# Loading queries, keys and values for two pairs of heads per transfer, in an attention and two-layer expert kernel

## The chip, the cores and the metric

The kernel runs on one core of a Trainium2 chip. The metric is the device time of one execution in microseconds (us); lower is better. Before the change it is 928.75 us, the median of 3 runs (927.66 to 928.97).

## The reference

Everything is float32. Attention over q, k, v of shape 4 x 8 x 576 x 64 has two branches whose results are added: one over rows averaged in fours, one over a band of seven neighbours. The result, as 2304 rows of 512, goes through two layers with weights 512 x 2048 and 2048 x 512, the first with an ELU, the second with `s * relu(h)^2 + b`.

```python
q_d, k_d, v_d = (x.reshape(B, H, Sd, 4, D).mean(axis=3) for x in (q, k, v))
out_up = np.repeat(softmax_attn(q_d, k_d, v_d), 4, axis=2)
scores = np.where(abs(i - j) < 4, scale * q @ k.T, -1e9)
out_local = softmax(scores) @ v
x = (out_up + out_local).transpose(0, 2, 1, 3).reshape(B * S, H * D)
x = elu(x @ w_in0) @ w_out0
x = (s * relu(x @ w_in1) ** 2 + b) @ w_out1
```

## The kernel before

Two heads make a pair; there are 16 pairs (4 batches times CH = 4 pairs, called slots u), numbered i = 4n + u. Their arrays are laid out by the host: q and k with the head's 64 features ahead of the 576 positions, v with the two heads of a pair side by side.

The program has two stages. The **attention stage** takes the pairs one by one (`pairs` makes a loop over three batches and the fourth batch written out), and the **layers** then work through 6 blocks of 384 rows in each of two layers, with 16 chunks of weights each. Weights come through two staging buffers (`wstage`) and are split into a high and a low part by ScalarE (`hi_w`) and GpSimd (`lo_w`); the first four chunks of layer 0 are loaded and split during attention.

Within attention the engines run as a pipeline, each with its own written-out order, held together by counting semaphores. For pair i:

- SyncE (`sync`, L236) issues every load. `load_qk` (L238) is 3 transfers: keys of both heads into `kall[:, u]` (128 partitions), and each head's queries into its half of the partitions of `qbd`. `load_v` (L245) is 7 transfers: 9 overlapping windows of 70 rows into `vwin`, as six transfers in pieces of 512 B, and the rows grouped in fours into `v4` (in profile rows: `v`).
- TensorE (`tensor`, L418) in step i: pooled scores of i + 1 (`dscores`, L435), four of the transposes of i (`turn`, L450), the band scores of pair **i + 2** (`scores`, L426), the other transposes, and then `values` of i (L470, L479). It works strictly in this order, so a late query or key of i + 2 holds back the values of i.
- GpSimd (`gpsimd`, L324) in step i: pooled queries of pair **i + 3** (`pool_q`, L364, L366), pooled values of i + 1 (`pool_v`, L371, L373), and in slots 1 and 3 the low part of a chunk of weights (L378).
- ScalarE (`scalar`, L558) and VectorE (`vector`, L675): exponentials, copies out of PSUM, masks, maxima, normalisation. ScalarE also takes the high part of a chunk (L586) in step 1 and 3 of each batch, in the middle of its other work.

SyncE begins with q, k of pair 0, of pair 1, v of 0, q, k of 2, v of 1, q, k of 3, v of 2. Then `step` (L280) runs for each i: it waits until the scores and the pooled sums of i have been made, issues q and k of pair i + 4 into the same slot, in slot 0 issues two chunks of weights after waiting for the split of the chunks before them, then waits for the values of pair i - 1 and issues v of pair i + 3:

```python
if left >= CH:                       # q, k of pair i + 4
    sp.wait_ge(scores_ready, i + 1); sp.wait_ge(q_pooled, i + 1); sp.wait_ge(k_pooled, i + 1)
    load_qk(n + 1, u)
if u == 0:                           # two chunks of weights
    ...
if left >= 3:                        # v of pair i + 3
    sp.wait_ge(values_ready, i + 1)
    load_v(n + (u + 3) // CH, (u + 3) % CH)
```

(`values_ready` starts at 1.) Loads go to one queue and are served in the order of their issue.

Of the kernel before, what the change touches and what calls it, by code (L numbers as in the profile page):

```python
# [27 lines left out]
def attention_moe_moe2(nc, q_t, k_t, v, w_in0, w_out0, w_in1, w_out1, s, b, out):  # L28
    B, H, D, S = q_t.shape
# [34 lines left out]
    with ExitStack() as whole:  # L64
# [19 lines left out]
        with ExitStack() as first:  # L84
# [37 lines left out]
        q_loaded = [sem(f"q_loaded{i}") for i in range(CH)]  # L122
        k_loaded = [sem(f"k_loaded{i}") for i in range(CH)]
        v_loaded = [sem(f"v_loaded{i}") for i in range(CH)]
        w_loaded = [[sem(f"w_{x}_loaded{i}") for i in range(2)] for x in ("in", "out")]
        sb_loaded = sem("sb_loaded")

# [44 lines left out]
        block = whole.enter_context(nc.Block())  # L172

# [63 lines left out]
        def _(sp):  # L237
            def load_qk(bb, slot):  # L238
                sp.dma_start(kall[:, slot, :],
                             k_t[bb, 2 * slot:2 * slot + 2].rearrange("h d s -> (h d) s")).then_inc(k_loaded[slot], 16)  # L240
                for h in range(2):
                    rows = slice(h * D, (h + 1) * D)
                    sp.dma_start(qbd[rows, slot, h, :], q_t[bb, 2 * slot + h]).then_inc(q_loaded[slot], 16)  # L243

            def load_v(bb, slot):  # L245
                vp = v[bb, slot]
                inner = vp[QT - REACH:QT - REACH + (NT - 2) * QT].rearrange("(t r) x -> r t x", r=QT)
                rest = vp[2 * QT - REACH:2 * QT - REACH + (NT - 2) * QT].rearrange("(t r) x -> r t x", r=QT)
                dst = vwin[:, slot].rearrange("p t h d -> p t (h d)")
                sp.dma_start(dst[0:QT, 1:NT - 1, :], inner).then_inc(v_loaded[slot], 16)  # L250
                sp.dma_start(dst[QT:WIN, 1:NT - 1, :], rest[0:2 * REACH]).then_inc(v_loaded[slot], 16)
                for t in (0, NT - 1):
                    a = WSTART[t]
                    sp.dma_start(dst[0:QT, t, :], vp[a:a + QT]).then_inc(v_loaded[slot], 16)
                    sp.dma_start(dst[QT:WIN, t, :], vp[a + QT:a + WIN]).then_inc(v_loaded[slot], 16)
                sp.dma_start(v4[:, slot].rearrange("p k i x -> p k (i x)"),
                             vp.rearrange("(k p i) x -> p k (i x)", k=2, i=POOL)
                             ).then_inc(v_loaded[slot], 16)
# [66 lines left out]
        def _(pool):  # L325
# [35 lines left out]
            def pool_q(n, u):  # L361
                pool.wait_ge(q_loaded[u], 32 * (n + 1))
                x = qbd[:, u].rearrange("p h (a i) -> p (h a) i", i=POOL)
                pool.tensor_tensor(q_half[:, u % 2], x[:, :, 0:2], x[:, :, 2:4], ALU.add).then_inc(q_part, 1)  # L364
# [3 lines left out]
            def pool_v(n, u):  # L368
                pool.wait_ge(v_loaded[u], 16 * NV * (n + 1))
                x = v4[:, u]  # L370
# [48 lines left out]
        def _(pe):  # L419
            def scores(n, u):  # L420
                pe.wait_ge(k_loaded[u], 16 * (n + 1))
                pe.wait_ge(q_loaded[u], 32 * (n + 1))
                for t in range(NT):
                    bank, a = (0, t * WIN) if t < NTA else (1, (t - NTA) * WIN)
                    for h in range(2):
                        mm = pe.matmul(ps_s[h * QT:(h + 1) * QT, bank, a:a + WIN], qbd[:, u, h, t * QT:(t + 1) * QT],  # L426
# [32 lines left out]
            def values(n, u):  # L459
                i = n * CH + u  # L460
                slot = u % 2
                pe.wait_ge(v_loaded[u], 16 * NV * (n + 1))
                pe.wait_ge(x_ready, i + 1)

                def band_tiles(tiles):
                    for t in tiles:
                        for h in range(2):
                            rows = slice(h * D, (h + 1) * D)
                            o = ps_x[rows, 0, t * QT:(t + 1) * QT] if t < NTA else ps_x[rows, 1, (t - NTA) * QT:(t - NTA + 1) * QT]
                            mm = pe.matmul(o, vwin[:, u, t, h, :], probt[:, t, h * QT:(h + 1) * QT], start=True, stop=True)  # L470
# [373 lines left out]
```

## Time and profile before

| | |
|---|---|
| median of 3 runs | 928.75 us |
| the profiled execution: its own time | 932.17 us |
| its span, first to last instruction | 930.4 us |
| attention stage | 0 to about 125 us of the span |
| TensorE busy over the span | 905.8 us (97%) |
| bytes read from HBM | 36.09 MB |

The span is 1.8 us shorter than the execution's own time, and that is 3.4 us over the median of the three runs. Times in rows count from the start of the span. A busy engine is an engine with an instruction under way; "idle before" gives the time an instruction's engine stood still and what released it. "SPq" is SyncE's issuing of transfers.

### The profile page before, as it was taken

What the parts mean: (1) busy time and instruction counts of PE and PEld (TensorE: products, weight loads), DVE (VectorE), ACT (ScalarE), POOL (GpSimd) and SP (SyncE); (2) the same over time, 40 slices, a digit from 0 to 9 for tenths busy, and PEclk for the clock granted to TensorE, in tenths of its full rate; (3) what the DMA queues carried; (4) which work ended last, traced back from release to release, by engine and by line L of the source; (5) the groups of instructions that cost most, each with busy time, mean ns of one, the idle gap of its engine ahead of it and who ended that gap; (6) DMA issues with size and microseconds to landing.
All of it is one profiled execution on the core that took longest, in us unless ns stands there. A gap on an engine that the chain in (4) does not pass through costs nothing.

```text
span 930.4 us, 16164 instructions
## 1 busy us (share of the span) xinstructions
PE 905.8 (97%) x5936; PEld 853.6 (92%) x5936; DVE 396.3 (43%) x774; ACT 413.1 (44%) x1104; POOL 148.3 (16%) x148
## 2 busy tenths in 40 slices
PE   5898999999999999999999999999999999999998
PEld 5777789999999999999999989899998999999896
DVE  6788844233233233232333453443443443443433
ACT  8889976544344343344466432232232332322222
POOL 5565647300000000000156400000000000000000
PEclk9889999999999999999999999999999999999999
DMA  8987534200000000000044200000000000000000
GB/s 196 206 199 195 131 100 135 62 1 1 1 0 0 0 0 0 0 1 1 23 125 125 69 1 0 35 1 1 35 0 0 34 0 0 35 1 1 34 1 35
DMA packets 42929, 41.47 MB, mean 45 GB/s; under 512 B 3616, under 2 KB 30080, under 8 KB 42880
## 3 DMA queue, kind: packets, MB, share of 16 engines
q1 hardware_dynamic: 42880, 40.83, 16.7%
q8 instruction: 30, 0.49, 0.2%
q14 instruction: 19, 0.16, 0.1%
HBM read 36.09 MB, written 4.72 MB: 44 GB/s over the span
## 4 chain that ended last, share of the span: by engine, by line
PE 90%; SPq 2%; issue 2%; POOL 2%; DVE 2%; ACT 1%; DMA 1%; POOLq 0%; ACTq 0%; DVEq 0%
PE ps_h L517 43%; PE ps_y L538 22%; PE ps_y L536 21%; PE ps_t L450 1%; PE ps_sd L435 1%; POOL v L371 1%; SPq L243 1%; PE ps_xd L479 1%; PE ps_s L426 1%; ACT prob L568 1%; DMA wstage<-in_w_in 1%; PE ps_x L470 1%; DVE prob L700 0%; POOL q_half L364 0%; POOL qd L366 0%
## 5 line engine op out<-in xcount | busy, mean ns | idle before, releaser
L660 ACT ACTIVATE g_hi<-tmp 128x384 fp32r<-128x384 f32 x192 | 101.0, 526 | 262.5 <-PE ps_y L538 153.1
L654 ACT ACTIVATE tmp<-ps_h 128x384 f32<-128x384 f32 x192 | 94.2, 490 | 227.2 <-PE ps_h L517 224.7
L804 DVE TENSOR_TENSOR g_lo<-tmp,g_hi 128x384 fp32r<-128x384 f32 x192 | 107.4, 559 | 205.4 <-ACT g_hi L660 205.4
L517 PE MATMUL ps_h<-xs_hi,win_late_lo 128*128 128x384 f32 x576 | 193.8, 336 | 0.0
L517 PE MATMUL ps_h<-xs_hi,win_late_hi 128*128 128x384 f32 x576 | 193.8, 336 | 0.0
L517 PE MATMUL ps_h<-xs_lo,win_late_hi 128*128 128x384 f32 x576 | 193.6, 336 | 0.0
L796 DVE SCALAR_TENSOR_TENSOR tmp<-tmp,ps_h 128x384 f32<-128x384 f32 x96 | 53.2, 554 | 162.1 <-ACT tmp L657 161.2
L517 PEld LDWEIGHTS ps_h<-xs_lo,win_late_hi 128*128 128x128 f32 x576 | 108.3, 188 | 3.3
L517 PEld LDWEIGHTS ps_h<-xs_hi,win_late_hi 128*128 128x128 f32 x576 | 108.3, 188 | 3.2
L517 PEld LDWEIGHTS ps_h<-xs_hi,win_late_lo 128*128 128x128 f32 x576 | 108.3, 188 | 0.0
L800 DVE TENSOR_TENSOR tmp<-tmp 128x384 f32<-128x384 f32 x96 | 55.2, 575 | 121.1 <-ACT tmp L654 121.1
L536 PE MATMUL ps_y<-g_hi,wout_late_lo 128*128 128x384 f32 x288 | 96.8, 336 | 0.0
L536 PE MATMUL ps_y<-g_lo,wout_late_hi 128*128 128x384 f32 x288 | 96.8, 336 | 0.0
L536 PE MATMUL ps_y<-g_hi,wout_late_hi 128*128 128x384 f32 x288 | 96.8, 336 | 0.0
L538 PE MATMUL ps_y<-wout_late_hi,g_lo 128*128 128x512 f32 x216 | 85.2, 394 | 0.0
L538 PE MATMUL ps_y<-wout_late_lo,g_hi 128*128 128x512 f32 x216 | 85.0, 394 | 0.0
L538 PE MATMUL ps_y<-wout_late_hi,g_hi 128*128 128x512 f32 x216 | 84.9, 393 | 0.0
L517 PE MATMUL ps_h<-xs_hi,win_early_hi 128*128 128x384 f32 x192 | 64.7, 337 | 0.2 <-DVE xs_lo L749 0.2
L517 PE MATMUL ps_h<-xs_hi,win_early_lo 128*128 128x384 f32 x192 | 64.4, 335 | 0.0
L517 PE MATMUL ps_h<-xs_lo,win_early_hi 128*128 128x384 f32 x192 | 64.3, 335 | 0.0
L378 POOL TENSOR_TENSOR win_early_lo<-wstage,win_early_hi 128x512 fp32r<-128x512 f32 (+1 forms) x8 | 10.2, 1280 | 292.3 <-ACT win_early_hi L586 292.3
L536 PEld LDWEIGHTS ps_y<-g_lo,wout_late_hi 128*128 128x128 f32 x288 | 54.1, 188 | 0.0
(87 smaller groups left out, 1435.9 us busy)
## 6 DMA issues: line engine op xcount, KB each, us to landing
wstage<-in_w_in SPq DMA_DIRECT2D x32, 256.0 KB, 2.8
wstage<-in_w_out SPq DMA_DIRECT2D x32, 256.0 KB, 2.8
kall<-in_kt SPq DMA_DIRECT2D x16, 288.0 KB, 4.4
qbd<-in_qt SPq DMA_DIRECT2D x32, 144.0 KB, 4.2
v<-in_v SPq DMA_DIRECT2D x16, 288.0 KB
out<-wstage SPq DMA_DIRECT2D x18, 256.0 KB, 2.2
vwin<-in_v SPq DMA_DIRECT2D x16, 224.0 KB
vwin<-in_v SPq DMA_DIRECT2D x32, 32.0 KB
```

Source lines behind the costliest of these rows:

```text
L243: sp.dma_start(qbd[rows, slot, h, :], q_t[bb, 2 * slot + h]).then_inc(q_loaded[slot], 16)
L371: pool.tensor_tensor(x[:, :, 0:2, :], x[:, :, 0:2, :], x[:, :, 2:4, :], ALU.add).then_inc(v_part, 1)
L378: pool.tensor_tensor(lo, wstage[slot][:, half, :], hi.bitcast(F32), ALU.subtract).then_inc(w_split[half], 1)
L426: mm = pe.matmul(ps_s[h * QT:(h + 1) * QT, bank, a:a + WIN], qbd[:, u, h, t * QT:(t + 1) * QT], kall[:, u, WSTART[t]:WSTART[t] + WIN], sta ...
L517: mm = pe.matmul(o, w_chunk(0, a, j)[:, c * P:(c + 1) * P], xs[x][:, slot, c, :], start=(c == 0 and p == 0), stop=(c == CH - 1 and p == 2))
L536: mm = pe.matmul(ps_y[:, c, 0:TB], w_chunk(1, a, j)[:, c * P:(c + 1) * P], g[x][:, j % 2, :], **go)
L538: mm = pe.matmul(ps_y[:, c, 0:DM], g[a][:, j % 2, c * P:(c + 1) * P], w_chunk(1, x, j), **go)
L654: act.activation(x, ps_h[:, j % 4, 0:TB], ACT.Relu, scale=-1.0 if layer == 0 else 1.0).then_inc(relu_ready, 1)
L660: act.activation(g[0][:, j % 2, :], x, ACT.Copy).then_inc(hi_ready, 1)
L796: dve.scalar_tensor_tensor(out=x, in0=x, scalar=-1.0, in1=ps_h[:, j % 4, 0:TB], op0=ALU.add, op1=ALU.max).then_inc(act_ready, 1)
L800: dve.tensor_tensor(x, x, x, ALU.mult).then_inc(square_ready, 1)
L804: dve.tensor_tensor(g[1][:, j % 2, :], x, g[0][:, j % 2, :].bitcast(F32), ALU.subtract).then_inc(g_ready, 1)
```

## The change

Two pairs (slots 2g and 2g + 1) form a group. The host lays q, k and v out so that what a group needs of one partition lies together, and each transfer now brings both pairs: runs of 4608 B in place of 2304 B for q and k, 1024 B in place of 512 B in the windows of v, 4096 B in place of 2048 B in `v4`. There is one semaphore for each group's q, k and v in place of one for each slot. Pairs 0 and 1 alone still get q and k in transfers of their own, with two extra semaphores for pair 0. The other loads of q and k and all loads of v go by groups: the first ones come in the order q, k of 0; q, k of 1; v of 0 and 1; q, k of 2 and 3; v of 2 and 3. In `step`, q, k of the next batch's group are issued in slots 1 and 3 only (pairs i + 3 and i + 4), and so is v (the same two pairs, after the values of pair i).

```diff
-            qbd = sba("qbd", [P, CH, 2, S])
+            qbd = sba("qbd", [P, 2, CH, S])
             kall = sba("kall", [P, CH, S])
-            vwin = sba("vwin", [WIN, CH, NT, 2, D])
-            v4 = sba("v4", [KD, CH, 2, POOL, 2 * D])
+            vwin = sba("vwin", [WIN, CH // 2, NT, 2, 2, D])
+            v4 = sba("v4", [KD, CH // 2, 2, POOL, 2, 2 * D])
...
+        def wait_q(eng, n, u):
+            if isinstance(n, int) and n == 0 and u == 0:
+                eng.wait_ge(first_q_loaded, 32)
+            else:
+                eng.wait_ge(q_loaded[u // 2], 32 * (n + 1))
...
-            def load_qk(bb, slot):
-                sp.dma_start(kall[:, slot, :],
-                             k_t[bb, 2 * slot:2 * slot + 2].rearrange("h d s -> (h d) s")).then_inc(k_loaded[slot], 16)
+            def load_qk(bb, grp, a, z):
+                slots = slice(2 * grp + a, 2 * grp + z)
+                k_done, q_done = (first_k_loaded, first_q_loaded) if z == 1 else (k_loaded[grp], q_loaded[grp])
+                sp.dma_start(kall[:, slots, :], k_t[bb, grp, :, a:z, :]).then_inc(k_done, 16)
                 for h in range(2):
                     rows = slice(h * D, (h + 1) * D)
-                    sp.dma_start(qbd[rows, slot, h, :], q_t[bb, 2 * slot + h]).then_inc(q_loaded[slot], 16)
+                    sp.dma_start(qbd[rows, h, slots, :], q_t[bb, grp, h, :, a:z, :]).then_inc(q_done, 16)
...
-            load_qk(0, 0)
-            load_qk(0, 1)
+            load_qk(0, 0, 0, 1)
+            load_qk(0, 0, 1, 2)
             load_v(0, 0)
-            load_qk(0, 2)
+            load_qk(0, 1, 0, 2)
             load_v(0, 1)
-            load_qk(0, 3)
-            load_v(0, 2)
...
             def step(n, u, left):
                 i = n * CH + u
-                if left >= CH:
+                if left >= CH and u % 2 == 1:
                     sp.wait_ge(scores_ready, i + 1)
                     sp.wait_ge(q_pooled, i + 1)
                     sp.wait_ge(k_pooled, i + 1)
-                    load_qk(n + 1, u)
+                    load_qk(n + 1, u // 2, 0, 2)
                 if u == 0:
                     for half in range(2):
                         sp.wait_ge(w_split[half], n + 1)
                         load_w(0, n, half, 0)
-                if left >= 3:
-                    sp.wait_ge(values_ready, i + 1)
-                    load_v(n + (u + 3) // CH, (u + 3) % CH)
+                if left >= CH and u % 2 == 1:
+                    sp.wait_ge(values_ready, i + 2)
+                    load_v(n + 1, u // 2)
```

The consumers change only in their indices and in the semaphore they wait for.

**Order on SyncE, the first loads.** Each row is one instruction: its line, and the tile it fills with the shape (partitions first). Before, the loads of v of pair 0, q and k of pair 2, and the beginning of v of pair 1:

```order
L256 DMA v<-in_v 72x2x512
L239 DMA kall<-in_kt 128x576
L243 DMA qbd<-in_qt 64x576 x2
L250 DMA vwin<-in_v 64x7x128
L251 DMA vwin<-in_v 6x7x128
```

Now, the same place:

```order
L275 DMA v<-in_v 72x2x1024
L259 DMA kall<-in_kt 128x1152
L262 DMA qbd<-in_qt 64x1152 x2
L269 DMA vwin<-in_v 64x7x256
L270 DMA vwin<-in_v 6x7x256
```

The transfers are as many, and each is twice as large; the queries and keys of pair 2 stand behind the values of two pairs, and are complete only with those of pair 3.

**Order on SyncE, the first step of the loop** (`ISA` stands for register work and waits, `wstage` for a chunk of weights). Before, after the last of the first loads:

```order
L278 DMA sb<-in_b 128x1
L176 UNCONDITIONAL_BRANCH
L176 ISA
L239 ISA
L239 DMA kall<-in_kt 128x576
L243 DMA qbd<-in_qt 64x576
L243 ISA
L243 DMA qbd<-in_qt 64x576
L264 ISA
L264 DMA wstage<-in_w_in 128x4x128
L264 ISA
L264 DMA wstage<-in_w_out 128x512
```

Now:

```order
L295 DMA sb<-in_b 128x1
L192 UNCONDITIONAL_BRANCH
L192 ISA
L283 ISA
L283 DMA wstage<-in_w_in 128x4x128
L283 ISA
L283 DMA wstage<-in_w_out 128x512
L300 ISA
L259 ISA
L259 DMA kall<-in_kt 128x1152
L262 DMA qbd<-in_qt 64x1152
L262 ISA
```

The queries and keys of pair 4, which stood ahead of the first weights, now stand behind them and come together with those of pair 5.

## Rows read from the trace of the kernel before

**Rows 1.** Busy time by stretch, attention and layers; in brackets instruction counts.

```profile
core 0: us, PE busy (x) PEld busy (x) DVE busy (x) ACT busy (x) POOL busy (x), PEclk, DMA share, GB/s
0.00:125.00 125.00, 105.22 (x1621) 92.02 (x1622) 100.15 (x231) 109.86 (x500) 74.32 (x92) 0.90 0.73 173
125.00:930.40 805.40, 800.55 (x4317) 761.62 (x4315) 296.18 (x545) 303.20 (x604) 73.96 (x56) 1.00 0.08 25
```

**Rows 2.** Waits in 0:125 us: waiter, releaser, us in total, times, longest us.

```profile
PE ps_s L426 <- DMA qbd<-in_qt: 5.9, 1, 5.9
...
POOL q_half L364 <- DMA qbd<-in_qt: 1.6, 3, 1.1
ACT win_early_hi L586 <- DMA wstage<-in_w_in: 1.5, 1, 1.5
...
POOL v L371 <- DMA v<-in_v: 1.2, 1, 1.2
```

**Rows 3.** Chain that ended last, 8:60 us: start us, us, what.

```profile
22.21 5.62 DMA wstage<-in_w_in
27.95 0.10 ACT win_early_hi L586
...
33.54 1.23 PE ps_xd L479 x8
```

**Rows 4.** Busy time by stretch, the columns of rows 1; the clock at half.

```profile
36.00:40.00 4.00, 4.00 (x32) 3.38 (x32) 2.10 (x5) 2.33 (x11) 3.43 (x4) 0.50 0.96 216
```

**Rows 5.** DMA view, 0:28 us.

```profile
DMA packets 5556, 5.62 MB, mean 201 GB/s; under 512 B 827, under 2 KB 3713, under 8 KB 5552
...
q1 hardware_dynamic: 5552, 5.57, 89.4%
```

**Rows 6.** DMA view, 13:18 us.

```profile
DMA packets 851, 1.00 MB, mean 200 GB/s; under 512 B 108, under 2 KB 484, under 8 KB 851
...
q1 hardware_dynamic: 851, 1.00, 101.8%
```

**Rows 7.** DMA view, 23:28 us.

```profile
DMA packets 1388, 1.14 MB, mean 229 GB/s; under 512 B 112, under 2 KB 1108, under 8 KB 1386
```

**Rows 8.** DMA view, 130:930 us: source and target, count, KB each, us to landing.

```profile
wstage<-in_w_in SPq DMA_DIRECT2D x26, 256.0 KB, 2.7
wstage<-in_w_out SPq DMA_DIRECT2D x26, 256.0 KB, 2.8
```

**Rows 9.** DMA view, 28.5:30 us: the loads of pair 5.

```profile
kall<-in_kt SPq DMA_DIRECT2D x1, 288.0 KB, 5.2
qbd<-in_qt SPq DMA_DIRECT2D x2, 144.0 KB, 4.7
```

**Rows 10.** Instructions of SyncE in order of time.

```profile
28.75 1.18 SPq L243 DMA_DIRECT2D qbd<-in_qt  x2
...
78.25 0.34 SPq L264 DMA_DIRECT2D wstage<-in_w_out  x1
```

**Rows 11.** Instructions of TensorE in order of time.

```profile
16.47 1.33 PE L426 MATMUL ps_s<-kall,qbd 128*64 128x70 f32 x36
...
28.89 1.33 PE L426 MATMUL ps_s<-kall,qbd 128*64 128x70 f32 x36
30.97 0.30 PE L450 MATMUL ps_t<-ident,prob 128*70 128x128 f32 x1 [0.75 <-ACT probt L612]
...
70.91 0.64 PE L470 MATMUL ps_x<-probt,vwin 70*64 70x64 f32 x16
```

**Rows 12.** Instructions of GpSimd in order of time.

```profile
13.52 1.14 POOL L364 TENSOR_TENSOR q_half<-qbd 128x576 f32<-128x576 f32 x1 [0.37 <-DMA qbd<-in_qt]
...
27.88 1.15 POOL L364 TENSOR_TENSOR q_half<-qbd 128x576 f32<-128x576 f32 x1 [2.03 <-DVE probd L743]
...
31.07 0.73 POOL L373 TENSOR_TENSOR vd<-v 72x256 f32<-72x256 f32 x1
...
85.75 1.15 POOL L364 TENSOR_TENSOR q_half<-qbd 128x576 f32<-128x576 f32 x1 [1.90 <-DVE probd L743]
```

More of the change, by code:

```diff
@@ L28, in attention_moe_moe2 @@
 def attention_moe_moe2(nc, q_t, k_t, v, w_in0, w_out0, w_in1, w_out1, s, b, out):
-    B, H, D, S = q_t.shape
+    B, GROUPS, _, D, _, S = q_t.shape
+    H = 4 * GROUPS
     DM, F = w_in0.shape
@@ L119, in attention_moe_moe2 @@
             ps_y = second.enter_context(nc.psum_tensor("ps_y", [P, 4, 512], F32))
-        q_loaded = [sem(f"q_loaded{i}") for i in range(CH)]
-        k_loaded = [sem(f"k_loaded{i}") for i in range(CH)]
-        v_loaded = [sem(f"v_loaded{i}") for i in range(CH)]
+        q_loaded = [sem(f"q_loaded{i}") for i in range(CH // 2)]
+        k_loaded = [sem(f"k_loaded{i}") for i in range(CH // 2)]
+        v_loaded = [sem(f"v_loaded{i}") for i in range(CH // 2)]
         w_loaded = [[sem(f"w_{x}_loaded{i}") for i in range(2)] for x in ("in", "out")]
         sb_loaded = sem("sb_loaded")
+        first_k_loaded = sem("first_k_loaded")
+        first_q_loaded = sem("first_q_loaded")
         pads_zero = sem("pads_zero")
@@ L172, in attention_moe_moe2, with wait_k @@
         block = whole.enter_context(nc.Block())
+        def wait_k(eng, n, u):
+            if isinstance(n, int) and n == 0 and u == 0:
+                eng.wait_ge(first_k_loaded, 16)
+            else:
+                eng.wait_ge(k_loaded[u // 2], 16 * (n + 1))
+        def wait_q(eng, n, u):
+            if isinstance(n, int) and n == 0 and u == 0:
+                eng.wait_ge(first_q_loaded, 32)
+            else:
+                eng.wait_ge(q_loaded[u // 2], 32 * (n + 1))
         def pairs(eng, body):
@@ L361, in pool_q @@
             def pool_q(n, u):
-                pool.wait_ge(q_loaded[u], 32 * (n + 1))
-                x = qbd[:, u].rearrange("p h (a i) -> p (h a) i", i=POOL)
-                pool.tensor_tensor(q_half[:, u % 2], x[:, :, 0:2], x[:, :, 2:4], ALU.add).then_inc(q_part, 1)
+                wait_q(pool, n, u)
+                x = qbd[:, :, u, :].rearrange("p h (a i) -> p h a i", i=POOL)
+                half = q_half[:, u % 2].rearrange("p (h a) i -> p h a i", h=2)
+                pool.tensor_tensor(half, x[:, :, :, 0:2], x[:, :, :, 2:4], ALU.add).then_inc(q_part, 1)
                 pool.wait_ge(q_part, n * CH + u + 1)
@@ L420, in scores @@
             def scores(n, u):
-                pe.wait_ge(k_loaded[u], 16 * (n + 1))
-                pe.wait_ge(q_loaded[u], 32 * (n + 1))
+                wait_k(pe, n, u)
+                wait_q(pe, n, u)
                 for t in range(NT):
@@ L469, in band_tiles @@
                             o = ps_x[rows, 0, t * QT:(t + 1) * QT] if t < NTA else ps_x[rows, 1, (t - NTA) * QT:(t - NTA + 1) * QT]
-                            mm = pe.matmul(o, vwin[:, u, t, h, :], probt[:, t, h * QT:(h + 1) * QT], start=True, stop=True)
+                            mm = pe.matmul(o, vwin[:, u // 2, t, u % 2, h, :], probt[:, t, h * QT:(h + 1) * QT], start=True, stop=True)
                     return mm
@@ L594, in _ @@
                     rows = slice(h * D, (h + 1) * D)
-                    act.activation(qbd[rows, slot, 1 - h, :], ident[rows, 0:1].broadcast_to([D, S]),
+                    act.activation(qbd[rows, 1 - h, slot, :], ident[rows, 0:1].broadcast_to([D, S]),
                                    ACT.Copy, scale=0.0).then_inc(slots_zero, 1)
@@ L822, with lay_k, lay_v @@
     from concourse.bass_utils import run_bass_kernel_spmd
+    def lay_k(k):
+        x = k.reshape(k.shape[0], -1, 2, 2, *k.shape[2:]).transpose(0, 1, 3, 5, 2, 4)
+        return np.ascontiguousarray(x).reshape(*x.shape[:2], -1, *x.shape[4:])
+    def lay_v(v):
+        x = v.reshape(v.shape[0], -1, 4, *v.shape[2:]).transpose(0, 1, 3, 2, 4)
+        return np.ascontiguousarray(x).reshape(*x.shape[:3], -1)
     nc = bacc.Bacc("TRN2", target_bir_lowering=False, num_devices=1)
     arrays = {
-        "in_qt": np.ascontiguousarray(q.transpose(0, 1, 3, 2)),
-        "in_kt": np.ascontiguousarray(k.transpose(0, 1, 3, 2)),
-        "in_v": np.ascontiguousarray(v.reshape(v.shape[0], v.shape[1] // 2, 2, *v.shape[2:]).transpose(0, 1, 3, 2, 4)).reshape(
-            v.shape[0], v.shape[1] // 2, v.shape[2], 2 * v.shape[3]),
+        "in_qt": np.ascontiguousarray(q.reshape(q.shape[0], -1, 2, 2, *q.shape[2:]).transpose(0, 1, 3, 5, 2, 4)),
+        "in_kt": lay_k(k),
+        "in_v": lay_v(v),
         "in_w_in0": np.ascontiguousarray(moe_w_in),
```

30 lines of the change are left out of this document (15 added, 15 removed).

## The prediction

> **What bounds the kernel now.** I read the busy time by stretch first. From 125 us on TensorE is busy 800.55 of 805.40 us at full clock [rows 1]: the layers are bound by TensorE, and the transfers there (25 GB/s, a share of 0.08) are nothing to it. The change does not touch them, so whatever it gains or loses in the attention stage is added to the end one for one, as long as it moves the first layer. The attention stage is bound by no engine alone: in 125 us TensorE is busy 105.22, VectorE 100.15, ScalarE 109.86 [rows 1]; each works in its fixed order and the chain passes from one to the next. A stall at one place shifts all that follows.
>
> Second, the waits: who waits for a transfer? TensorE once, 5.9 us, for the first queries; GpSimd three times 1.6 us together for queries and once 1.2 us for values; ScalarE once 1.5 us for the first chunk of weights [rows 2]. All lie in the first 28 us; after that loads come in time. The chain of waits shows that only the start matters: through the weights, issued at 22.21 and waited for by ScalarE at 27.95, to TensorE's pooled values of pair 2 at 33.54 [rows 3].
>
> Third, the transfers themselves. Up to 28 us the queue holds the DMA engines at 89.4% of their time, 5.62 MB at 201 GB/s [rows 5], and from 13 to 18 us at 101.8% [rows 6]. So in this stretch **what decides when something arrives is the number of bytes that stand ahead of it**. This is what the change alters.
>
> **The change, part by part.**
>
> *Bytes.* None are saved. A pair has 576 KB of queries and keys (288 and twice 144 [rows 9]), 0.590 MB, and, by the shapes of its seven transfers, 603 KB of values, 0.617 MB. A weight chunk is twice 256 KB [rows 8], 0.524 MB.
>
> *Longer runs.* Does the rate rise with them? From 13 to 18 us the engines handled 851 packets at 200 GB/s [rows 6], from 23 to 28 us 1388 packets, mostly of 512 B, at 229 GB/s [rows 7]: more and shorter packets, and not slower. And 256 KB of `w_in`, read in runs of 512 B, land 2.7 us after issue, 256 KB of `w_out` in runs of 2048 B 2.8 us [rows 8]. By these rows runs of twice the length are worth nothing. The queue was not quite full, though (89.4%), and the issuing of half as many transfers closes that gap: up to 28 us at the rate of a full queue, 201 / 0.894 = 225 GB/s, would be some 10% more. Bounds: 0 and 10%; I take the middle, 5%, since the stretch from 13 to 18 us was full and still moved only 200 GB/s. The Trainium skill, "DMA: Bandwidth & Descriptors", section Bandwidth, says to batch transfers to 1 MiB or more, and gives 138 GB/s for one of 64 KB and 341 GB/s for one of 1 MB. By it the stage would be fed far faster; the rows above, with many transfers in flight at once, show no such growth.
>
> *Issuing on SyncE.* Ten issues for two pairs in place of twenty. No row shows an engine waiting for a load after 28 us [rows 2], so this is worth nothing there.
>
> *Queries of pair 2.* Before they stood behind 3 pairs of q, k and 1 of v, with their own: 2.39 MB, and GpSimd took them at 13.52 [rows 12]. Now they are complete with q, k of 4 pairs and v of 2: 3.59 MB. At 212 GB/s (201 with 5% more) the 1.20 MB more are 5.7 us, so 19 us. TensorE wanted them at 16.47 [rows 11]: 2 to 3 us late. Part of this is covered: ScalarE stands still 1.5 us for weights before 27.95 [rows 2, 3], and the weights have the same bytes ahead of them as before (5.07 MB then, 5.09 now). What is left is about 1 us, and the next stall is later and larger, so the two don't add.
>
> *Queries of pair 4.* This is the main term. Before they came ahead of the first weights, 4.79 MB. Now they follow v of pair 3, the weights, and come complete with those of pair 5: 6 pairs of q, k, 4 of v and one chunk, 3.54 + 2.47 + 0.52 = 6.53 MB. That is to within 0.01 MB what stood ahead of the queries of pair **5** before, and those were issued from 28.75 to 29.93 [rows 10] and landed a median of 4.7 us later [rows 9]: 34 us. With the transfers 5% faster, counted from their start at about 1.5 us, 34 - 0.05 x 32.5 = 32.4, and with the bounds 30.8 to 34. TensorE wanted them at 28.89 and the scores took 1.33 [rows 11]. The next instruction, the transposes at 30.97, itself waited 0.75 for ScalarE [rows 11], so the scores of pair 4 could end there without loss. They now end at 32.4 + 1.3 = 33.7, the transposes are held until then, and behind them the values of pair 2 on TensorE, then the copies and exponentials on ScalarE, and pair 4's mask on VectorE: **+2.7 us**, with bounds +1.2 and +4.4. On GpSimd the pooled queries of pair 4 (27.88 [rows 12]) wait as well, and pair 2's pooled values, done at 31.07 + 0.73 = 31.8 [rows 12], stand behind them and move by 32.4 - 27.88 = 4.5 to 36.3. TensorE took them at 33.54 [rows 3], so 36.3 is late by 2.8: the same price, not a second one.
>
> *Later batches.* Queries of a group are issued after the second chunk of weights. For pairs 12 and 13 that is after 78.25 [rows 10]; ahead stand v of pairs 10 and 11, issued once the values of pair 7 are done, 70.91 + 0.64 [rows 11], so from about 72 on. Together 1.23 + 0.52 + 1.18 = 2.94 MB at 212 GB/s = 13.9 us, so 86, and GpSimd wants the queries at 85.75 [rows 12]. The slack there is about nothing. Bounds 0 and 1.5 us at each of two places (pairs 8 and 12). I take 0.3 in all.
>
> *Operands in another layout.* GpSimd's and TensorE's reads are as many elements with other strides. The nearest rows of two shapes on GpSimd are 1.15 us for 576 elements and 0.73 us for 256 [rows 12], 2.0 and 2.9 ns each; so between nothing and, with 0.9 ns on 576 elements, 0.5 us a pair, of which only what is on the chain counts. I take 0, since the innermost runs stay as long as they were.
>
> The sum: 2.7 + 0.3 = **+3.0 us**. The profiled execution took 932.17, its span 930.4; with +3.0 the span would be 933.4, the own time 935.2. This execution was 3.4 us over the median, so against the median: 928.75 + 3.0 = 931.8.
>
> **The rivals.**
>
> *Rival 1: the cover holds, no difference.* If the full queue with longer runs moves 225 GB/s or more from the start, the queries of pair 4 are there by 30 or so, and the loss is under 1.9 us. For it: the 89.4% [rows 5]. Against: 101.8% of engine time at 200 GB/s [rows 6]. Time 929.5. Chance 0.25.
>
> *Rival 2: faster.* If the rate grows by a quarter (250 GB/s), pair 4's queries are complete at 1.5 + 32.5 / 1.25 = 27.5, before TensorE wants them, and the weights arrive at 22 to 23 in place of 27.95. ScalarE's 1.5 us go [rows 2]. Besides, TensorE's clock fell to the half level (0.50 from 36 to 40 us [rows 4]), just after ScalarE and then TensorE had stood still; without that stall it might stay up; TensorE's 4.00 busy us there would be 2 at full clock, of which some 1.5 may reach the end. Total -1.5 to -3: 926. It decides from about 20% more GB/s. It is what the Trainium skill's rule of large transfers would make of this kernel. Against it speak all of rows 6 to 8. Chance 0.14.
>
> *Rival 3: late loads again and again.* If bursts of 1.2 MB make GpSimd wait at pairs 8 and 12, and the later stall lets the clock fall to the half level once more, 1.5 us twice and 1.5 us for the clock come on top of 3.0: 936. For it: the slack worked out above. Chance 0.11.
>
> *The change does not do what it says* can be left out: the shapes on SyncE's rows are twice as large.
>
> **How the numbers follow.** The forecast, queries of pair 4 late by 1.9 to 4.5 us in all, has 0.50; rival 1 0.25, rival 2 0.14, rival 3 0.11. A difference of 0.2%, 1.86 us, is about what a measurement of this kernel can tell. Slower by more: 0.50 + 0.11 = 0.61, rounded down to 0.59 because the lower bound of the main term lies under 1.86. Same: 0.27. Faster: 0.14. The likeliest case is 931.8. The range runs from 927.0, which takes in rival 1 and the mild part of rival 2, to 936.5, which takes in most of rival 3.
>
> **What would show it.** In the changed kernel's profile: TensorE's scores of pair 4, with a wait for queries that ends at 31 to 34 us; GpSimd's pooled queries of the same pair waiting for a transfer of some 4 us; the scores of pair 2 at about 19; no wait of ScalarE for weights; the first instructions of the layers some 3 us later; half as many packets of q, k and v, and GB/s up to 28 us under 225. I am wrong if the queries of pair 4 are there before 30 us (the rate grew), or if the first layer begins no later in spite of that wait (something else gave the time back).

## The result and the profile after

| | before | changed |
|---|---|---|
| time, median | 928.86 us (927.66 to 932.24) | 940.05 us (938.0 to 943.09) |
| ratio to before | | 1.0132, 95% interval 1.0104 to 1.0159 |
| profiled execution, own time / span | 932.17 / 930.4 us | 941.33 / 939.5 us |
| first product of the first layer begins | 124.07 us | 133.21 us |

Slower by 11.2 us, where 3.0 were forecast: the sign held, the size did not, and the time lies outside the range of 927.0 to 936.5. In both profiles 806.3 us pass from the first product of the layers to the end of the span, so the whole loss is in the attention stage, as the prediction's first step had it. The loss of the two profiles is 9.1 us; the rest of the 11.2 is that the profiled execution of the kernel before was itself 3.3 over its median, and that of the changed kernel 1.3. Ratios, and the comparison by clock further down, leave out executions that the record counts as slow; medians take in all.

By windows (columns: stretch, its length, busy time of TensorE, its weight loads, VectorE, ScalarE, GpSimd with their instructions, granted TensorE clock, DMA share, GB/s) the changed kernel shows, beside [rows 1] and [rows 4]:

```profile
0.00:125.00 125.00, 100.36 (x1510) 88.73 (x1511) 93.44 (x218) 102.78 (x473) 69.34 (x89) 0.89 0.79 172
125.00:939.50 814.50, 808.86 (x4429) 768.56 (x4426) 301.93 (x556) 310.87 (x633) 78.57 (x60) 1.00 0.08 24
```

```profile
12.00:16.00 4.00, 1.25 (x8) 1.24 (x7) 3.64 (x9) 4.00 (x25) 0.38 (x1) 0.86 1.04 190
16.00:20.00 4.00, 2.15 (x10) 1.46 (x9) 1.52 (x3) 2.63 (x12) 1.75 (x2) 0.71 1.07 214
20.00:24.00 4.00, 3.32 (x53) 2.88 (x55) 1.75 (x4) 1.07 (x6) 1.81 (x2) 0.71 1.13 211
24.00:28.00 4.00, 4.00 (x46) 3.88 (x43) 2.73 (x8) 2.98 (x17) 1.60 (x2) 0.50 1.12 173
28.00:32.00 4.00, 4.00 (x46) 3.38 (x44) 1.43 (x3) 2.53 (x10) 2.16 (x3) 0.51 0.81 231
```

The layers run as before. In the first 125 us every engine does less, GpSimd too. From 24 to 32 us TensorE is at the half level (0.50 and 0.51) and has no idle time left; in the 4 us from 16 it had worked 2.15. In windows of half a microsecond the trace has two stretches at the half level here, 14.9 to 18.3 and 21.7 to 31.9 us. The first begins before any query is late, after TensorE had stood idle from about 12.0 to 14.8; the kernel before stood idle there even longer (3.57 us, to 14.64) and kept the full clock. So only the second can be put down to the late queries. Before, it was at 0.50 from 36 to 40 us [rows 4], and below the full clock in several later windows too (0.57 from 64 to 68, for one). Over the whole stage the difference is small: by the trace's clock TensorE is at the half level for 23.9 us of the attention stage before, and for 30.7 in the changed kernel. If it worked all through them, the 6.8 us more cost 3.4, an estimate and an upper one.

Who waits for a transfer? The waits of the first 137 us (engine, line, buffer, releaser: us in all, times, the longest), to be read against [rows 2]:

```profile
POOL q_half L382 <- DMA qbd<-in_qt: 15.9, 6, 4.6
...
PE ps_s L444 <- DMA qbd<-in_qt: 10.1, 3, 6.1
```

GpSimd's waits for queries were 1.6 us, three times, all in the first 14 us. Now they are 15.9 us, and they go on through the whole stage. There is no wait of ScalarE for weights. The instructions of GpSimd in order of time (start, duration, idle time before it and what ended that):

```profile
15.62 1.41 POOL L389 TENSOR_TENSOR v<-v 72x512 f32<-72x512 f32 x1 [5.50 <-DMA v<-in_v]
20.80 1.15 POOL L382 TENSOR_TENSOR q_half<-qbd 128x576 f32<-128x576 f32 x1 [2.96 <-DMA qbd<-in_qt]
36.31 1.15 POOL L382 TENSOR_TENSOR q_half<-qbd 128x576 f32<-128x576 f32 x1 [6.07 <-DVE probd L761]
50.47 1.14 POOL L382 TENSOR_TENSOR q_half<-qbd 128x576 f32<-128x576 f32 x1 [3.44 <-DMA qbd<-in_qt]
68.16 1.15 POOL L382 TENSOR_TENSOR q_half<-qbd 128x576 f32<-128x576 f32 x1 [3.46 <-DMA qbd<-in_qt]
97.48 1.15 POOL L382 TENSOR_TENSOR q_half<-qbd 128x576 f32<-128x576 f32 x1 [4.58 <-DMA qbd<-in_qt]
```

These are the values of pair 0 and the queries of pairs 2, 4, 6, 8 and 12. The one at 36.31 (pair 4, the prediction's main term) is not a wait for a load: VectorE released it, since all before it was already late. TensorE's own rows:

```profile
20.68 1.49 PE L444 MATMUL ps_s<-kall,qbd 128*64 128x70 f32 x36 [2.54 <-DMA qbd<-in_qt]
29.95 2.25 PE L444 MATMUL ps_s<-kall,qbd 128*64 128x70 f32 x36
49.12 0.58 PE L488 MATMUL ps_x<-probt,vwin 70*64 70x64 f32 x6 [3.24 <-issue]
97.45 1.33 PE L444 MATMUL ps_s<-kall,qbd 128*64 128x70 f32 x36 [1.44 <-DMA qbd<-in_qt]
```

The start of TensorE's scores, pair by pair, gives the loss its places:

| pair | 2 | 3 | 4 | 5 | 6 | 8 | 10 | 12 | 15 |
|---|---|---|---|---|---|---|---|---|---|
| before, us | 16.5 | 22.4 | 28.9 | 39.0 | 45.3 | 59.3 | 73.4 | 88.5 | 106.7 |
| changed, us | 20.7 | 29.9 | 36.7 | 43.3 | 54.9 | 69.3 | 83.5 | 97.5 | 117.2 |
| later by | 4.2 | 7.5 | 7.8 | 4.3 | 9.6 | 10.0 | 10.2 | 9.0 | 10.5 |
| second profile (*after_again*), later by | 4.0 | 8.1 | 8.3 | 4.8 | 6.4 | 7.6 | 5.7 | 5.7 | 6.7 |

4.2 us are lost at pair 2. 3.3 more come by pair 3, whose scores take 2.25 us at the half clock where [rows 11] has 1.33 at the full one. Between pairs 4 and 5 some of it comes back, since the kernel before had its own stretch of half clock there [rows 4]. Then pair 6 is later again, by 5.3: its queries come late, and 3.24 us are a stall of TensorE in the middle of the values of pair 3, which the trace puts down to nothing ("issue"). A 16 KB transfer of instructions begins in that gap, at 46.2 us, so a late instruction fetch is my reading of it, argued and not shown; in a second profile of the same program the stall is absent, and pair 6 is only 1.6 us later than pair 5 was. In neither profile does the lateness grow much from pair 6 on, though GpSimd waits at pairs 8 and 12: what an engine waits is not what the kernel loses.

The chain of waits (start, duration, what) begins with

```profile
8.89 11.74 DMA qbd<-in_qt
20.68 1.49 PE ps_s L444 x36
```

where [rows 3] had 22.21 for a weight chunk. And the transfers up to 28 us, beside [rows 5]:

```profile
DMA packets 3422, 5.44 MB, mean 194 GB/s; under 512 B 592, under 2 KB 2260, under 8 KB 3420
...
q1 hardware_dynamic: 3420, 5.42, 97.5%
...
kall<-in_kt SPq DMA_DIRECT2D x2, 576.0 KB, 12.3
qbd<-in_qt SPq DMA_DIRECT2D x4, 288.0 KB, 12.3
```

38% fewer packets, each longer, and **not more bytes a second**: 194 GB/s with the engines' time filled to 97.5%, where it was 201 at 89.4%. From 13 to 18 us it is 189 GB/s at 104.1%, against 200 at 101.8% [rows 6].

When did the queries of pair 4 arrive in this kernel? SyncE issued them with pair 5's, and the DMA view of that stretch (18.5 to 22.6 us) gives the time to landing:

```profile
18.78 1.26 SPq L259 DMA_DIRECT2D kall<-in_kt  x1
20.14 2.30 SPq L262 DMA_DIRECT2D qbd<-in_qt  x2
...
kall<-in_kt SPq DMA_DIRECT2D x1, 576.0 KB, 14.3
qbd<-in_qt SPq DMA_DIRECT2D x2, 288.0 KB, 13.0
```

So they landed at 33 to 34 us, near the upper bound of the prediction (32.4, at most 34), and no engine was there to wait for them.

What happens later, when the first burst is over? SyncE's transfers from 34 us on:

```profile
34.99 0.63 SPq L269 DMA_DIRECT2D vwin<-in_v  x1
...
38.57 0.32 SPq L275 DMA_DIRECT2D v<-in_v  x1
39.22 0.36 SPq L259 DMA_DIRECT2D kall<-in_kt  x1
39.72 1.30 SPq L262 DMA_DIRECT2D qbd<-in_qt  x2
```

Values of pairs 4 and 5 first, the queries and keys of 6 and 7 right behind. GpSimd gets these queries at 50.47. The DMA view from 35 to 50.4 us:

```profile
DMA packets 1159, 2.45 MB, mean 159 GB/s; under 512 B 126, under 2 KB 756, under 8 KB 1156
...
q1 hardware_dynamic: 1156, 2.42, 71.9%
```

2.4 MB in 15.4 us. The queue starts empty, SyncE needs 6 us to issue it all, and a completion now stands for two pairs. The 159 GB/s are a mean over the whole wait: from 35 to 37 us 38 GB/s moved, from 37 to 47 us 205, and from 49 to 50.4 us 30. It is the beginning and the end of the burst that are slow, not its middle.

### The profile page after: what moved, and what is told of

Same layout as the page of the kernel before. It is cut to its first block, busy times and chain, and to the rows that moved or that the text cites. A ratio compares the mean times of both kernels' runs of the same rounds, so it can differ in the third digit from the quotient of the medians.

```text
span 939.5 us, 15979 instructions
## 1 busy us (share of the span) xinstructions
PE 909.2 (97%) x5936; PEld 857.3 (91%) x5936; DVE 395.4 (42%) x774; ACT 413.6 (44%) x1104; POOL 147.9 (16%) x148
## 4 chain that ended last, share of the span: by engine, by line
PE 90%; POOL 2%; issue 2%; DVE 2%; DMA 1%; SPq 1%; ACT 1%; POOLq 0%; DVEq 0%; ACTq 0%
PE ps_h L535 43%; PE ps_y L556 21%; PE ps_y L554 21%; DMA qbd<-in_qt 1%; PE ps_t L468 1%; PE ps_s L444 1%; PE ps_x L488 1%; POOL v L389 1%; PE ps_sd L453 1%; PE ps_xd L497 1%; POOL q_half L382 1%; DVE prob L718 1%; POOL qd L384 0%; POOL vd L391 0%; ACT prob L586 0%
## 5 line engine op out<-in xcount | busy, mean ns | idle before, releaser
L396 POOL TENSOR_TENSOR win_early_lo<-wstage,win_early_hi 128x512 fp32r<-128x512 f32 (+1 forms) x8 | 10.2, 1280 | 292.3 <-ACT win_early_hi L604 292.3
```

What stands on the lines that cost most here:

```text
L396: pool.tensor_tensor(lo, wstage[slot][:, half, :], hi.bitcast(F32), ALU.subtract).then_inc(w_split[half], 1)
```

## The experiments

Each variant computes the whole of the reference. Besides its time I give for each what the waits of its trace show, and the time at which the first product of the layers begins: from there to the end all take 806.3 us (one 807.9), so it is the loss of one profile. Single executions scatter more than that (the eight of the changed kernel lie between 936.19 and 943.33 us); so ratios are given with their 95% intervals.

### Does it repeat?

*after_again*: the changed kernel, unedited.

> The changed kernel once more, beside the others. The profile of its first run showed a wait of 3.24 us of TensorE inside the values of pair 3 that no semaphore explains. If that is a chance event, this profile lacks it and the time is some 3 us less; if it belongs to the kernel, it is there again. Ratio to the kernel before 1.010 to 1.016.

Measured 939.92 us, 1.0121 (1.0074 to 1.0168); span 935.7, the layers from 129.38. GpSimd waits for queries 17.8 us in 7 places; the "issue" stall is gone. So the lateness of queries is a property of the program, and some 3 to 4 us of the first profile's 9.1 are of that execution alone. The half level here runs from 15.3 to 32.4 us without a break, so it begins 5 us before the wait for pair 2's queries; in all it is 30.7 us of the stage, as in the first profile.

### The runs, or the grouping?

*short_qk*: the changed kernel with 256 B of padding in device memory between the two pairs of each group, so that a run of queries or keys is one pair again (2304 B) and all else stays.

```diff
-kall, qbd <- in_kt, in_qt [.., pair, 576]        (4608 B in one run)
+kall, qbd <- in_kt, in_qt [.., pair, 576 of 640] (2304 B a run)
```

> The changed kernel, with 256 B of padding in HBM between the two pairs' queries and between their keys: the same transfers, sizes, order and waits, but runs of 2304 B in place of 4608 B. If the length of the runs is worth nothing: within 2 us of the changed kernel (940), and the same GB/s up to 28 us (194). If long runs help: slower, 943 or more. If long runs hold others up: 937 or less.

937.37 us, 1.0099 (1.0068 to 1.0131), first layer from 131.62. Up to 28 us:

```profile
DMA packets 3558, 5.32 MB, mean 190 GB/s; under 512 B 531, under 2 KB 2102, under 8 KB 3556
...
q1 hardware_dynamic: 3556, 5.30, 96.6%
```

Nothing is lost by halving the runs of queries and keys; the waits are the same (GpSimd 19.4 us for queries, 7 times). The median is 2.7 us under the changed kernel's, a little more than the 2 expected, but the two intervals overlap: a small gain from shorter runs is neither shown nor ruled out.

*group_short*: grouping and its order, but a long run nowhere. Queries and keys of two pairs come in one transfer of short runs, values in transfers of one pair, with one semaphore for each group; in SBUF the operands lie as in the kernel before.

```diff
-sp.dma_start(kall[:, slots, :], k_t[bb, grp, :, a:z, :])
+sp.dma_start(kall[:, slots, :], k_t[bb].rearrange("(g h) d s -> (h d) g s", h=2)[:, slots, :])
...
-    vp = v[bb, grp]
+for slot in (2 * grp, 2 * grp + 1):
+    vp = v[bb, slot]
```

> The changed kernel's order, waits and group semaphores, with the layouts of the kernel before: q and k of two pairs in one transfer but in runs of 2304 B, v in one-pair transfers (14 for a group) in runs of 512 B and 2048 B. Theory A (the loss is the order: bytes ahead of the queries of pair 2 and of the later groups): within 2 us of the changed kernel, ratio 1.009 to 1.015. Theory B (long runs themselves are slow and hold up other transfers): the loss mostly gone, ratio under 1.005.

944.49 us, 1.0152 (1.0109 to 1.0194), first layer from 139.29. In its waits:

```profile
POOL q_half L380 <- DMA qbd<-in_qt: 23.8, 6, 7.7
```

The loss is there without any long run, so the runs don't cause it, nor do they heal it. Its rate up to 28 us is 200 GB/s at 87.4%, that of the kernel before. Set beside *short_qk* (190 at 96.6%), this puts the fuller engine time down to the values, whose transfers and runs are twice as large there and not here. And the loss is no smaller with the operands laid out as before, so their new layout is not its cause.

### The order alone

Three variants keep the transfers and the semaphores of one pair, as before, and change only the order of issue.

*order_single*: the order of the changed kernel throughout.

```diff
-q,k 0; q,k 1; v 0; q,k 2; v 1; q,k 3; v 2
+q,k 0; q,k 1; v 0; v 1; q,k 2; q,k 3; v 2; v 3
...
-if left >= CH:              load_qk(n + 1, u)
+if left >= CH and u % 2:    load_qk(n + 1, u - 1); load_qk(n + 1, u)
...
-if left >= 3:               load_v(n + (u + 3) // CH, (u + 3) % CH)
+if left >= CH and u % 2:    load_v(n + 1, u - 1); load_v(n + 1, u)
```

> The kernel before with its own transfers and one semaphore per pair, but issued in the order of the changed kernel, at the start and in the loop (slots 1 and 3). Against group_short it lacks only the waiting for a whole group. Theory A: the queries of pair 2 are there about 2.5 us sooner than with groups (0.6 MB less), so a third to a half of the loss is gone, ratio 1.004 to 1.009. Theory B: ratio under 1.003.

*start_only*: the first of these three edits, and in the loop one pair at each step (values of pair i + 4 after those of pair i are done). *loop_only*: the other two, with the first loads as before and values of pair 3 at their end.

> The kernel before, one pair a transfer, with the first loads in the changed kernel's order (v of pair 1 ahead of q, k of pair 2, v of pair 3 at the end); in the loop q, k of one pair and v of one pair in every step. Theory C: the start alone is worth 2 to 5 us, ratio 1.002 to 1.006, and no waits for queries after 40 us. If the start's order costs nothing: ratio under 1.002.

> The kernel before with its own first loads in their own order (v of pair 3 added at their end), but the loop issues two pairs at a time in slots 1 and 3 as the changed kernel does. Theory A, with the loss at the start: ratio 0.998 to 1.004, scores of pair 2 at about 16.5 us. If the loop's bursts are what costs (rival 3 of the prediction): ratio 1.006 or more, GpSimd waiting for queries in later batches.

| | median | ratio, interval | first layer from |
|---|---|---|---|
| order_single | 935.94 | 1.0092 (1.0056 to 1.0128) | 127.49 us |
| start_only | 936.61 | 1.0103 (1.0026 to 1.0179) | 125.64 us |
| loop_only | 940.58 | 1.0130 (1.0097 to 1.0163) | 129.89 us |

The order alone, with transfers of one pair, costs 0.9% where the changed kernel costs 1.3%. *order_single* came out at the upper end of what was expected; *start_only* (1.002 to 1.006 expected) and *loop_only* (0.998 to 1.004, if the start were all) lost more than the theory had, though the interval of *start_only* is wide. The waits lie where the edit is. *start_only*, GpSimd and ScalarE:

```profile
17.60 1.15 POOL L365 TENSOR_TENSOR q_half<-qbd 128x576 f32<-128x576 f32 x1 [3.96 <-DMA qbd<-in_qt]
...
31.09 0.63 ACT L587 ACTIVATE win_early_hi<-wstage 128x512 f32 x1 [3.56 <-DMA wstage<-in_w_in]
```

*loop_only*, GpSimd at pairs 4, 8 and 12, then TensorE at pair 4:

```profile
33.70 1.15 POOL L367 TENSOR_TENSOR q_half<-qbd 128x576 f32<-128x576 f32 x1 [5.21 <-DMA qbd<-in_qt]
62.24 1.15 POOL L367 TENSOR_TENSOR q_half<-qbd 128x576 f32<-128x576 f32 x1 [3.67 <-DMA qbd<-in_qt]
91.90 1.15 POOL L367 TENSOR_TENSOR q_half<-qbd 128x576 f32<-128x576 f32 x1 [4.79 <-DMA qbd<-in_qt]
```

```profile
33.68 1.33 PE L429 MATMUL ps_s<-kall,qbd 128*64 128x70 f32 x36 [2.08 <-DMA qbd<-in_qt]
```

Here the start is on time, and the wait at pair 4 that the prediction foretold (31 to 34 us) stands in the open: 33.7. *order_single* has it at 32.12, with 2.47 us on TensorE.

It comes there by a path that is in part another. With one pair in a transfer SyncE has twice as many to issue, and values of pair 3 have joined the first loads. Queries of pair 4 are issued at 20.16 us before, but only at 25.83 in *loop_only* and at 27.36 in *order_single*, where the changed kernel issues them at 20.14. From 24 to 28 us the DMA share in *loop_only* is 0.79: the queue was not full, and the bytes ahead alone did not decide. So these variants show that such an order costs about as much, and not that every microsecond of the changed kernel is lost in the same way. Nor do the parts add: either half of the order costs about what the whole does, and the three intervals overlap. One edit is in both halves, values of pair 3 ahead of the queries of pair 4. Whether that explains it wasn't tried.

### Curing one place

*qk_ahead*: the changed kernel, its transfers and first loads, but in the loop the queries and keys of a group go ahead of the values of the group before.

```diff
-w; q,k(4,5); v(4,5); q,k(6,7); v(6,7); w; q,k(8,9); v(8,9); q,k(10,11)
+w; q,k(4,5); q,k(6,7); v(4,5); q,k(8,9); v(6,7); w; q,k(10,11); v(8,9)
```

> The changed kernel with the same grouped transfers and the same first loads, but in the loop SyncE issues the queries and keys of a group ahead of the values of the group before it, as soon as their buffers are free. Theory C (two losses: the start, and in every later group queries that stand behind a burst of values): GpSimd's waits for queries after the first 28 us (3.4 to 4.6 us each, at pairs 6, 8 and 12) are gone, the loss of the start stays; ratio 1.004 to 1.008 against 1.013 for the changed kernel. Theory D (grouping as such costs, wherever it is issued): within 2 us of the changed kernel.

935.98 us, 1.0078 (1.0051 to 1.0104), first layer from 125.37. As expected of two losses, the start and the loop. In its waits:

```profile
POOL v L402 <- DMA v<-in_v: 6.6, 1, 6.6
POOL q_half L395 <- DMA qbd<-in_qt: 4.4, 3, 3.0
```

No wait for queries is left after 28 us; the longest is 2.95 us at 21.68. So **queries behind a burst of values cost the changed kernel about 4 us**, which the prediction had priced at 0.3; the start keeps about 7. The 7 are what is left over, not the result of curing the start alone.

*qk_ahead_first*: and queries and keys of pairs 2 and 3 ahead of the values of pairs 0 and 1 in the first loads.

> As qk_ahead, and at the start the queries and keys of pairs 2 and 3 go ahead of the values of pairs 0 and 1. They then have 2.36 MB before them as in the kernel before (2.39), so the scores of pair 2 run at about 16.5 again; the values of pair 0 are complete only after 3.59 MB, at 19 to 20 us, and TensorE takes them 2 to 3 us late. Theory C (what is left is the start): ratio 1.001 to 1.005. Theory D: ratio 1.006 or more, as qk_ahead.

937.37 us, 1.0099 (1.0066 to 1.0132), first layer from 128.52: a miss (1.001 to 1.005 was expected). The scores of pair 2 begin at 17.8, and now the values are late:

```profile
22.11 1.27 POOL L402 TENSOR_TENSOR v<-v 72x512 f32<-72x512 f32 x1 [12.19 <-DMA v<-in_v]
```

In a full queue something must be last. The order before, one pair of each in turn, brings each thing when it is wanted; in portions of two pairs neither of the two orders tried here does.

*loop_ahead*: can both places be cured while the loop still issues two pairs together? Transfers of one pair, first loads as in *loop_only*, loop as in *qk_ahead*.

> Transfers of one pair with semaphores of one pair and the first loads in the order of the kernel before, with values of pair 3 at their end; then the weights, and from there two pairs at a time with the queries and keys of a group ahead of the values of the group before. Theory A (the whole loss is two places: loads of the start grouped, and queries of later groups behind values): both are gone here, so 927 to 930.5, no wait for queries after 28 us, and the scores of pair 4 begin before 32. Rival (issuing two pairs at once costs by itself, by bursts that delay whatever stands behind them, in whatever order): values or keys are waited for in the loop and it takes 933 to 938.

938.53 us, 1.0074 (1.0037 to 1.0111), first layer from 131.30: a miss. (The plain ratio of the two medians, 938.53 to 929.0, is 1.0103; either way it is slower.) GpSimd, then ScalarE:

```profile
33.48 1.15 POOL L378 TENSOR_TENSOR q_half<-qbd 128x576 f32<-128x576 f32 x1 [5.51 <-DMA qbd<-in_qt]
```

```profile
30.29 0.63 ACT L600 ACTIVATE win_early_hi<-wstage 128x512 f32 x1 [1.92 <-DMA wstage<-in_w_in]
62.15 0.63 ACT L600 ACTIVATE win_early_hi<-wstage 128x512 f32 x1 [4.75 <-DMA wstage<-in_w_in]
```

The first row I should have foreseen. Values of pair 3 and the weights stand ahead of pair 4's queries again, 5.94 MB with their own (pair 5's stand behind them here), SyncE issues them only at 25.02, and they come at 33.5, as in *loop_only*. In the loop it is the rival's case: with queries and keys ahead, the weights are behind the bursts, and ScalarE waits 4.75 us for them. A wait moved from queries to weights.

### The clock

*after_warm*: the changed kernel with 12 products more on TensorE, whose results nothing uses, before its first scores.

```diff
+for _ in range(12):
+    pe.matmul(ps_xd[:, 0:P], ident[:], ident[:], start=True, stop=True)
```

> The changed kernel with 12 more matmuls of TensorE (128x128 by 128 columns, into a PSUM tile not yet in use) ahead of its first step, in time in which it waits for ScalarE. They add no result. In the changed kernel TensorE runs at its half clock level from 21.7 to 31.9 us. If that is a cost of its own on top of the late queries, it shrinks or goes here and the time falls by 1 to 3 us. If the late queries alone set the pace, the time stays within 1 us.

938.79 us, 1.0118 (1.0056 to 1.018), first layer from 130.97. The half clock still held from 19.3 to 33.0 us: the added products ran from 10.8 to 13.7, and the clock fell in the idle time that came after, before the scores of pair 2:

```profile
21.29 0.97 PE L444 MATMUL ps_s<-kall,qbd 128*64 128x70 f32 x12 [4.92 <-DMA qbd<-in_qt]
```

It separates nothing: neither what the half clock costs by itself nor whether late queries alone set the pace.

The record separates more than this run. Beside each time it has the mean clock granted in that execution. Ten executions of the kernel before had 0.982 to 0.985, and their median is 934.3 us; seven of the eight of the changed kernel lie in the same band, with a median of 941.3. So about 7 us are lost at an equal mean clock, and some 4 of the 11 go with the lower clock of the changed kernel. These are executions sorted afterwards and not an experiment, but they fit the 3.4 us that the half level can have cost in the profiles.

### Against the kernel before

*weights_first*: the kernel before, with the weights of a step issued ahead of that step's queries, keys and values, since its one late wait after the first loads is ScalarE's 1.5 us for weights [rows 2].

```diff
-q,k(n + 1, u); if u == 0: w(n); v
+if u == 0: w(n); q,k(n + 1, u); v
```

> The kernel before with one swap: in slot 0 the two chunks of weights are issued ahead of the queries and keys of the next batch. The weights have 0.59 MB less ahead of them, so ScalarE's wait of 1.50 us at 27.95 goes, and the queries of pair 4 come 2.4 us later, at about 28, just as TensorE wants them. By the rule that bytes ahead decide: 0 to 3 us faster than before, ratio 0.997 to 1.000.

> The same kernel as weights_first (the kernel before with the weights of a step issued ahead of the queries, keys and values of that step). Theory (those 1.5 us of waiting for weights are a true loss of the kernel before): again 926.5 to 928, 0.998 of before, and with both runs together the interval lies under 1. Rival (scatter of the start): 928.5 to 931.

*weights_first0*: the same for the first chunk alone, with SyncE's first round of the loop written out.

> The kernel before, with the first two chunks of weights ahead of the queries and keys of pair 4, and the later weights where they were, behind the queries (batch 0 written out on SyncE for it). In weights_first GpSimd waited 1.9 us for queries at pair 8; that wait is gone here. 1 to 3 us faster than before, ratio 0.997 to 0.999; scores of pair 4 at about 30, no wait for weights.

| | median | before, measured beside it | ratio, interval | first layer from |
|---|---|---|---|---|
| weights_first | 927.55 | 928.93 | 0.9977 (0.9945 to 1.0009) | 118.40 us |
| weights_first_again | 928.65 | 929.0 | 0.9983 (0.9957 to 1.001) | 120.04 us |
| weights_first0 | 933.93 | 928.52 | 1.0063 (1.0024 to 1.0101) | 120.60 us |

The wait for weights is gone in all three, and their profiled executions are 3.5 to 5.7 us shorter than that of before. But that one was itself 3.4 over its median, and both intervals of *weights_first* take in 1: no loss, and a gain of 0.2% that is not shown. Why *weights_first0* is slower, where a gain was expected, isn't settled. Its twelve executions run from 928.5 to 942.0; the five above 937 had a mean clock of 0.981 to 0.987, the seven others 0.988 to 0.991, and its profiled execution was a short one and shows no cause.

## Why the prediction was right or wrong

1. **"In this stretch what decides when something arrives is the number of bytes that stand ahead of it."** Right for the changed kernel, and by it the sign: its queries of pair 4 landed at 33 to 34 us, the upper bound, counted at the old rate. The rule needs a full queue, though. That they come at 33.7 and 33.5 in *loop_only* and *loop_ahead* as well is no second proof of it: there it is 5.94 MB and not 6.53, and SyncE issues them 5 us later than before.
2. **"Bounds: 0 and 10%; I take the middle, 5%"** for longer runs: wrong. Measured were 194 GB/s for 201, so 0 or a little less. The gap of 10% in the queue did close, to 97.5%, but with longer engine time for the same bytes and not with more bytes. [rows 6 to 8] had said so; the 5% were an argument against the rows. And more than half of the gap was never one: the 28 us of [rows 5] begin before the first transfer, and from 2 to 28 us the kernel before had a share of 0.96 at 215 GB/s (the changed one 1.04 at 208). The Trainium skill, "DMA: Bandwidth & Descriptors", section Bandwidth, says to batch transfers to 1 MiB or more; here transfers of 576 KB for 288 brought no rate, and queries took a median of 12.3 us from issue to landing in the first 28 us.
3. Queries of pair 2: **"2 to 3 us late. Part of this is covered"**, **"What is left is about 1 us, and the next stall is later and larger, so the two don't add."** This is the step that failed most: a term of the sum put at nothing, which held about 7 of the 11 us by what *qk_ahead* leaves. They came at 20.7 and not at 19, 4.2 us late: 3.59 MB at 194 GB/s from 1.5 us on is 20.0. And nothing covered it. The cover named, ScalarE's wait for weights, did vanish, but what stood behind it was later already. TensorE then worked at the half clock from 21.7 to 31.9 us, and pair 3's scores were 7.5 us late. The sum had no term for that clock; rival 3 priced it at 1.5 us, for a stall later on and not for one at 20 us.
4. Queries of pair 4, **"the main term"**, +2.7 us: the arrival was foretold well (33 to 34 us for 32.4), the wait was not. GpSimd and TensorE come to pair 4 late already (36.3 and 36.7), when the loads are there, so this term added nothing. Where the start is on time it is real: 2.08 us on TensorE at pair 4 in *loop_only*. That the forecast had the right sign it owes to other terms than the one it named.
5. Later batches, **"I take 0.3 in all."** Wrong in size. GpSimd waits 3.44, 3.46 and 4.58 us at pairs 6, 8 and 12, and *qk_ahead*, without these, is 4 us faster than the changed kernel. The sum used 212 GB/s, the rate of a full queue, from the moment of issue. At 212 the 2.41 MB ahead of pair 6 need 11.4 us; they took 15.4, since little moves in the first 2 us and in the last 1.4. And pair 6, where no weights stand between, was left out of the count.
6. Operands in another layout, taken at 0: right. GpSimd's 128x576 take 1.15 us as before [rows 12].
7. Rival 3 (late loads again and again, with another stretch of half clock, 936) was the nearest case and had 0.11. Its mechanism is one of the two found, and its price of 1.5 us a place not far off: GpSimd waited 3.4 to 4.6 us at each of three, but *qk_ahead* gives back about 4 in all. What it lacked is the start, for it was built on top of the 3.0. Rivals 1 and 2 both needed the rate to grow, and it did not.
8. Of the announced signs two held (under 225 GB/s, no wait for weights) and a third nearly (in the first 125 us 12538 packets for 21483, not half); pair 2's scores came at 20.7 for 19; the load waits at pair 4, on GpSimd and on TensorE, are missing; and the layers start 9 us later in this profile and 5.3 in the second, not 3.

What stays open: how the 11 us split exactly between late loads and the half clock (about 7 and 4 by the executions of equal clock), since no experiment held the clock fixed; what curing the start alone would give back, since no variant in portions of two pairs did so; and why the two halves of the order don't add up.

## What to carry to other kernels

In a queue that is full, as here, a larger portion was not a faster one: it makes everything behind it wait for the whole portion, and its own first part wait for its last. Cost a regrouping of loads by the bytes ahead of each consumer's first need, for every group and not only the first, and for a burst that starts with an empty queue add the time before its bytes flow. Ask too who issues the loads and when: a transfer that is issued late is late however few bytes stand ahead of it. And a small stall early in a chained stage isn't covered by a later wait unless what stands behind that wait was on time.

## What the runs showed of the hardware

- Packets 1.6 times as large on the mean did not raise the rate of a full queue: 5556 packets at 201 GB/s and 89.4% of the engines' time [rows 5], 3422 at 194 and 97.5%. Shortening only the queries' and keys' runs left it so (190, 96.6%); values of one pair in short runs gave the old figures (200, 87.4%).
- TensorE can stand still for 3.24 us in the middle of a group of 20 matmuls whose operands are all there (45.88 to 49.12). It came in one of two profiles of the same program, and a gap of the same kind, 1.03 us, in *qk_ahead*. The cause isn't shown.
- A queue whose engines are busy all the time has no one rate. Before, from 13 to 18 us, it is 200 GB/s at 101.8% [rows 6]; in *loop_only* from 28 to 30 us, with weights, queries and keys issued just before, it is nearly twice that:

```profile
DMA packets 427, 0.77 MB, mean 386 GB/s; under 512 B 55, under 2 KB 101, under 8 KB 425
...
q1 hardware_dynamic: 425, 0.75, 103.5%
```

- The half clock doesn't need a late load. From 16 to 20 us the granted clock was 0.50 in *loop_only* and 0.56 in *weights_first_again*, whose queries of pair 2 were on time; in the kernel before it was 1.00 there. With a late load behind it the stretch is longer: from 12 to 40 us the mean is 0.76 and 0.70 in the two profiles of the changed kernel, 0.88 before, 0.94 and 0.88 in the two of *weights_first*.
